# Attention and two feed-forward stages: scores four groups ahead, value spans in two transfers, first weights split in smaller parts

## The chip, the cores and the metric

The kernel runs on one core of a Trainium2 chip. The metric is the device time of one execution in microseconds (us); three runs of the kernel before gave a median of 616.96 us (616.08 to 617.96). The engines are TensorE (PE, its weight loads PEld), VectorE (DVE), ScalarE (ACT), GpSimd (POOL) and SyncE (SP), which issues nearly all transfers (DMA).

## The reference, cut to what matters

```python
# attention, B=2, H=8, S=768, D=64, block 32, band 16
k_sum = k.reshape(B, H, nb, 32, D).max(axis=3)
v_sum = v.reshape(B, H, nb, 32, D).mean(axis=3)
scores_l = where(|i - j| < 16, q @ k.T / sqrt(D), -1e9)
scores_s = q @ k_sum.T / sqrt(D) + log(32)
a = softmax(concat([scores_l, scores_s]))         # sum + 1e-9
x = a @ concat([v, v_sum])                        # -> 1536 tokens x 512
# two feed-forward stages, 512 -> 2048 -> 512
h = maximum(x @ w_in, 0);  x = (h * h) @ w_out
h = x @ w2_in;  g = P(h) / (Q(h) + 1e-6);  out = g @ w2_out
```

## The kernel before, in words

**Attention.** The 16 heads are 8 pairs (`NB`), and a pair's 768 queries are 12 windows of 64 queries, each with 96 keys and 24 block maxima (120 columns, `COLS`). Four windows of both heads make a group, so there are 24 groups G, three to a pair. A group goes through: `scores(G)` on PE; `masked(G)` on DVE (mask and row minimum, from PSUM into a buffer `prob`); `exps(G)` on ACT; `guard(G)` and `invert(G)` on DVE; `normalise(G)` on POOL; `turn(G)` on PE (transpose); a copy to `probT` on ACT; `output(G)` on PE. There are three `prob` buffers (`P_RING`), and PE runs the scores three groups ahead of the output. After every second group DVE splits the result into a high and a low part (`x_hi`, `x_lo`), since every product of the feed-forward stages is three products of such parts.

**Inputs of a pair.** q, kT (padded to 800 columns) and the value windows `vw` (96 rows of 12 x 128 numbers, 6 KB a row) come by one transfer each into rings of three buffers (`RING`). `block_max` on DVE makes the block maxima of the keys in three parts, one a group; POOL builds the key windows (`load_windows`, `spread_all`). `summary(n)` on PE makes the block means of the values, ACT copies them (`copy_summary`), and then SP spreads them by four small transfers into the rows 96 to 119 of the value windows (`spread_summary`); `output(3n)` waits for these.

**What sets the order.** Each engine runs one list written out by hand, with semaphores between them. SP issues in program order: a transfer that has to wait holds up all behind it. Before, iteration n of SP's loop issues the values of pair n+2, k and q of pair n+3 and a first weight slot, and then waits for the summary of pair n+1 (made on PE in group 3n) and spreads it.

**From attention to the first feed-forward stage.** The stage has 48 steps; a step is `hidden` (12 matmuls) and `sum_b` (12 matmuls), with `hidden` two steps ahead. `hidden(0)` and `hidden(1)` stand between the last groups, ahead of `output(22)` and `output(23)`. Their weights (three slots land early) have to be split first: slots 0 and 1 whole on DVE (`split`, after groups 22 and 23's softmax work), slot 2 by halves on POOL, beginning in group 20. Then come the second half of that stage and stage two (`chunk_c`), whose lists the change leaves alone.

Of the kernel before, what the change touches and what calls it, by code (L numbers as in the profile page):

```python
# [28 lines left out]
P = 128  # L29
# [25 lines left out]
DVE_FIRST = 2  # L55
# [6 lines left out]
P_RING = 3  # L62
RING = 3
NB = PAIRS * B
XPAIRS = GROUPS // 2
KP = S + 2 * BAND

# [11 lines left out]
def build(nc, qT, kT, vw, w1, w2, coef_a, coef_b, out):  # L79
# [50 lines left out]
    ksum = [places[1](f"ksum{r}", [P, NBLK]) for r in range(RING)]  # L130
    assert all(a.offset <= w + 2 * half for a, w in zip(places, (W_HI, W_LO)))
    area = Area(WORK)
    prob = [area(f"prob{i}", [P, GU, COLS]) for i in range(P_RING)]
    probT = [area(f"probT{i}", [COLS, GU * P]) for i in range(2)]
    mask = area("mask", [P, 3, COLS])
# [28 lines left out]

    q_in = [sem(f"q_in{r}") for r in range(RING)]
    k_in = [sem(f"k_in{r}") for r in range(RING)]
    vw_in = [sem(f"vw_in{r}") for r in range(RING)]
    vsum_in = [sem(f"vsum_in{r}") for r in range(RING)]
# [7 lines left out]
    means_done = sem("means_done")  # L176
# [24 lines left out]
    w_early, w_late = sem("w_early"), sem("w_late")  # L201
# [27 lines left out]
    def _(sp):  # L229
        def load_k(n):  # L230
            if n >= RING:
                sp.wait_ge(windows_ready, GPB * (n - RING + 1))
            sp.dma_start(kraw[n % RING][:, :], kT[n]).then_inc(k_in[n % RING], 16)
# [6 lines left out]
        def load_vwin(n):  # L240
            if n >= RING:
                sp.wait_ge(o_done, done(2, GPB * (n - RING + 1) - 1))
            sp.dma_start(vwin[n % RING][0:KW, :, :], vw[n]).then_inc(vw_in[n % RING], 16)

        def spread_summary(n):

            sp.wait_ge(vsum_copied, n + 1)
            for t in range(4):
                rows = KW + 2 * GPB * t
                sp.dma_start(vwin[n % RING][rows:rows + 2 * GPB, :, :],  # L250
                             vsum[n % 2][32 * t:32 * t + 2 * GPB, :].unsqueeze(1).to_broadcast([2 * GPB, NW, P])
                             ).then_inc(vsum_in[n % RING], 16)
# [17 lines left out]
        sp.dma_start(ca[:, :], coef_a.partition_broadcast(P)).then_inc(coef_in, 16)  # L270
        sp.dma_start(braw[:, :], coef_b.partition_broadcast(P)).then_inc(coef_in, 16)
        spread_summary(0)
        for n in range(NB):
            if n + 2 < NB:
                load_vwin(n + 2)
            if n + RING < NB:
                load_k(n + RING)
                load_q(n + RING)
            if 2 <= n < 2 + EARLY:
                load_first(n - 2)  # L280
            if n >= 5:
# [24 lines left out]
    def _(pool):  # L306
# [31 lines left out]
        def load_windows(n):  # L338

            pool.wait_ge(k_in[n % RING], 16 * (n // RING + 1))  # L340
# [30 lines left out]
        pool.wait_ge(k_in[0], 16)  # L371
        for gi in range(GPB):
            windows(0, GU * gi, GU * (gi + 1))
# [5 lines left out]
        spread_all(1)  # L379

        for G in range(GROUPS):
            n, gi = divmod(G, GPB)
            if G + 1 < GROUPS:
                normalise(G + 1, (G + 1) % P_RING)
            if n + 2 < NB:
# [4 lines left out]
            x = G - GROUPS + 4  # L390
            if x >= 0:
                if x == 0:
                    pool.wait_ge(w_first, 16 * EARLY)
                if x < 2 * (EARLY - DVE_FIRST):
                    split(half_slot(DVE_FIRST + x // 2, x % 2), w_hi_pool, x, w_early)

# [18 lines left out]
        for x in range(2 * LATE):  # L415
# [4 lines left out]
            split(half_slot(j, x % 2), w_hi_pool, 2 * (EARLY - DVE_FIRST) + x, w_late)  # L420
# [9 lines left out]
    def _(pe):  # L430
# [22 lines left out]
        def summary(n):  # L453

            pe.wait_ge(vw_in[n % RING], 16 * (n // RING + 1))
            pe.wait_ge(vsum_copied, n)
            for j in range(GPB):
                for t in range(4):
                    last = mm(vps[32 * t:32 * t + 32, 0:P], means[:, j, :], vwin[n % RING][0:KW, GPB * t + j, :],  # L459
# [11 lines left out]
        def output(G):  # L471
# [4 lines left out]
            if gi == 0:  # L476
                pe.wait_ge(vsum_in[r], 64 * (n // RING + 1))
# [515 lines left out]
```

## Time and profile before

| | us |
|---|---|
| median of 3 runs | 616.96 (616.08 to 617.96) |
| the profiled execution | 617.14 |
| its span, first to last instruction | 615.4 |
| PE busy | 582.0 (95%) |
| DVE busy | 444.0 (72%) |
| ACT busy | 261.3 (42%) |
| POOL busy | 145.1 (24%) |

The profiled execution lies 0.18 us above the median; 1.74 us of it lie around the span. Busy times are unions over an engine's instructions. The page cuts the span into 40 slices of 15.4 us: attention fills the first five, and the feed-forward stages all that follow.

### The profile page before, as it was taken

What the parts mean: (1) busy time and instruction counts of PE and PEld (TensorE: products, weight loads), DVE (VectorE), ACT (ScalarE), POOL (GpSimd) and SP (SyncE); (2) the same over time, 40 slices, a digit from 0 to 9 for tenths busy, and PEclk for the clock granted to TensorE, in tenths of its full rate; (3) what the DMA queues carried; (4) which work ended last, traced back from release to release, by engine and by line L of the source; (5) the groups of instructions that cost most, each with busy time, mean ns of one, the idle gap of its engine ahead of it and who ended that gap; (6) DMA issues with size and microseconds to landing.
All of it is one profiled execution on the core that took longest, in us unless ns stands there. A gap on an engine that the chain in (4) does not pass through costs nothing.

```text
span 615.4 us, 9725 instructions
## 1 busy us (share of the span) xinstructions
PE 582.0 (95%) x3360; PEld 472.8 (77%) x3360; DVE 444.0 (72%) x834; ACT 261.3 (42%) x553; POOL 145.1 (24%) x150
## 2 busy tenths in 40 slices
PE   4788699999999999999999989999999999999995
PEld 3556578888888888888888867788888888888884
DVE  4678787665343233456675699999999999999996
ACT  3778611111031111311111855556766566766564
POOL 5556610000030000210000656522221222221220
PEclk9999999999999999999999999999999999999999
DMA  8788433000000000022333200000100000100001
GB/s 232 212 261 251 129 128 148 0 1 0 1 0 0 0 0 0 0 81 91 103 102 103 69 1 0 1 0 1 68 0 0 0 0 0 68 1 0 1 2 68
DMA packets 12351, 32.68 MB, mean 53 GB/s; under 512 B 1568, under 2 KB 3872, under 8 KB 12320
## 3 DMA queue, kind: packets, MB, share of 16 engines
q1 hardware_dynamic: 12320, 32.25, 16.8%
q8 instruction: 21, 0.34, 0.2%
q14 instruction: 10, 0.08, 0.0%
HBM read 27.92 MB, written 3.15 MB: 50 GB/s over the span
## 4 chain that ended last, share of the span: by engine, by line
PE 47%; DVE 36%; issue 9%; ACT 3%; DMA 2%; DVEq 1%; POOL 1%; SPq 1%; POOLq 0%
PE bank L499 22%; PE bank L544 21%; DVE ratio L927 9%; DVE numer L909 6%; DVE ratio L921 5%; DVE numer L907 5%; DVE ratio L916 5%; DVE hhi L934 4%; ACT prob L617 2%; DMA vwin<-vsum 2%; PE bank L468 1%; PE bank L449 1%; PE bank L485 1%; PE bank L459 1%; SPq L250 1%
## 5 line engine op out<-in xcount | busy, mean ns | idle before, releaser
L499 PE MATMUL bank<-xhi,whi 128*128 (+1 forms) x384 | 150.3, 391 | 0.3 <-DVE wlo L820 0.3
L499 PE MATMUL bank<-xlo,whi 128*128 (+1 forms) x384 | 149.9, 390 | 0.0
L499 PE MATMUL bank<-xhi,wlo 128*128 (+1 forms) x384 | 149.8, 390 | 0.0
L630 ACT ACTIVATE hsq<-bank 128x512 f32<-128x512 f32 x48 | 28.8, 600 | 218.5 <-PE bank L499 218.5
L409 POOL TENSOR_TENSOR denom<-denom,habs 128x512 f32<-128x512 f32 (+1 forms) x49 | 62.3, 1272 | 250.9 <-ACT denom L686 250.9
L499 PEld LDWEIGHTS bank<-xhi,whi 128*128 128x128 f32 x384 | 72.5, 189 | 15.9 <-DVE wlo L820 0.7
L499 PEld LDWEIGHTS bank<-xhi,wlo 128*128 128x128 f32 x384 | 72.3, 188 | 15.1
L499 PEld LDWEIGHTS bank<-xlo,whi 128*128 128x128 f32 x384 | 72.4, 189 | 14.9
L559 PE MATMUL bank<-whi,hhi 128*128 128x512 f32 x192 | 75.9, 395 | 7.6 <-DVE hlo L938 7.6
L559 PE MATMUL bank<-whi,hlo 128*128 128x512 f32 x192 | 74.8, 390 | 0.0
L559 PE MATMUL bank<-wlo,hhi 128*128 128x512 f32 x192 | 74.8, 389 | 0.0
L544 PE MATMUL bank<-hhi,whi 128*128 128x512 f32 x192 | 74.7, 389 | 0.0
L544 PE MATMUL bank<-hlo,whi 128*128 128x512 f32 x192 | 74.7, 389 | 0.0
L544 PE MATMUL bank<-hhi,wlo 128*128 128x512 f32 x192 | 74.7, 389 | 0.0
L830 DVE TENSOR_TENSOR hsq<-hsq 128x512 f32<-128x512 f32 x48 | 33.5, 698 | 50.0 <-ACT hsq L630 49.8
L833 DVE TENSOR_SCALAR hhi<-hsq 128x512 fp32r<-128x512 f32 x48 | 21.1, 439 | 64.5 <-PE bank L544 64.3
L927 DVE SCALAR_TENSOR_TENSOR ratio<-numer,ca,ratio 128x512 f32<-128x512 f32 (+1 forms) x49 | 56.7, 1157 | 5.7
L401 POOL TENSOR_TENSOR xlo<-xraw,xhi 128x512 fp32r<-128x512 f32 x12 | 17.4, 1484 | 173.4 <-ACT xraw L663 173.4
L683 ACT ACTIVATE habs<-bank 128x512 f32<-128x512 f32 x48 | 28.8, 599 | 66.8 <-PE bank L499 51.6
L559 PEld LDWEIGHTS bank<-whi,hhi 128*128 128x128 f32 x192 | 36.0, 188 | 19.0 <-DVE hlo L938 11.8
L694 ACT ACTIVATE bank<-denom,one 128x512 f32<-128x512 f32 (+1 forms) x49 | 33.6, 686 | 32.3 <-POOL denom L409 32.3
L938 DVE TENSOR_TENSOR hlo<-ratio,hhi 128x512 fp32r<-128x512 f32 (+1 forms) x49 | 42.0, 858 | 1.7
(65 smaller groups left out, 858.9 us busy)
## 6 DMA issues: line engine op xcount, KB each, us to landing
wraw<-w SPq DMA_DIRECT2D x32, 512.0 KB, 4.1
vwin<-vw SPq DMA_DIRECT2D x8, 576.0 KB, 5.4
kraw<-kT SPq DMA_DIRECT2D x8, 400.0 KB, 6.0
q<-qT SPq DMA_DIRECT2D x8, 384.0 KB, 6.4
out<-osb SPq DMA_DIRECT2D x12, 256.0 KB, 2.1
vwin<-vsum SPq DMA_DIRECT2D x32, 36.0 KB
ca<-coef_a SPq DMA_DIRECT2D x1, 2.0 KB, 10.7
braw<-coef_b SPq DMA_DIRECT2D x1, 1.0 KB, 11.8
```

Source lines behind the costliest of these rows:

```text
L409: g.tensor_tensor(denom[:, i, cols], denom[:, i, cols], habs[:, i, cols], ALU.mult).then_inc(q_done, 1)
L499: last = mm(hps[j % 2][:, :], W[a][:, j, kt * P:(kt + 1) * P], X[b][:, kt, bass.ds(CH * c, CH)], start=k == 0, stop=k == 3 * KT - 1)
L544: last = mm(acc[dt][:, :], W[a][:, j, KT * P + dt * P:KT * P + (dt + 1) * P], HID[b][:, j % 2, :], start=j == 0 and i == 0, stop=j == FT - ...
L559: last = mm(acc[t][:, :], HID[a][:, j % 2, t * P:(t + 1) * P], W[b][:, j, KT * P:], start=j == 0 and i == 0, stop=j == FT - 1 and i == 2)
L694: a.activation(rcp0[bank][:, cols], denom[:, i, cols], ACT.Ln, bias=one[:, 0:1]).then_inc(ln_done, 1)
L830: d.tensor_tensor(hsq[:, i, :], hsq[:, i, :], hsq[:, i, :], ALU.mult).then_inc(sq_done, 1)
L907: d.tensor_tensor(numer[:, i, :], hps[i][:, :], numer[:, i, :], ALU.mult).then_inc(horner_done, 1)
L909: d.scalar_tensor_tensor(numer[:, i, :], numer[:, i, :], ca[:, 1:2], hps[i][:, :], ALU.subtract, ALU.mult).then_inc(h_free, 1)
L916: d.scalar_tensor_tensor(ratio[:, cols], denom[:, i, cols], one[:, 0:1], rcp0[bank][:, cols], ALU.add, ALU.mult).then_inc(t1_done, 1)
L921: d.scalar_tensor_tensor(ratio[:, cols], ratio[:, cols], -2.0, rcp0[bank][:, cols], ALU.add, ALU.mult).then_inc(t2_done, 1)
L927: d.scalar_tensor_tensor(ratio[:, cols], numer[:, i, cols], ca[:, 0:1], ratio[:, cols], ALU.subtract, ALU.mult).then_inc(ratio_done, 1)
L938: d.tensor_tensor(hlo[:, i, cols], ratio[:, cols], hhi[:, i, cols].bitcast(F32), ALU.subtract).then_inc(g_ready, 1)
```

## The change

- **Look-ahead.** Four `prob` buffers; PE runs the scores four groups ahead, ACT the exponentials three, DVE `guard` and `invert` and POOL `normalise` two groups ahead of `turn`, one more than before at each.
- **Values.** Four value buffers (`V_RING`); each value load is two transfers of 96 rows of 3 KB. `summary(n)` stands in group 3n-4 for n from 3 on, and in groups 0, 1 and 3 for n = 0, 1 and 2. SP's iteration n loads pair n+3 whole and then spreads pair n+2; ahead of the first spread it now also loads the values of pair 2 and the keys of pair 3.
- **Start.** The keys of pair 0 come in three parts, one of them issued by ACT; keys are no longer padded in memory, the edges are cleared on DVE; the copies that make `means` go from DVE to ACT.
- **First weights.** The w_in half of slots 0 to 2 is split on POOL in six quarter slots, one in each of the groups 17 to 22; the w_out half on DVE in groups 21 to 23. PE does `hidden(0)` and `hidden(1)` in eight pieces of three matmuls, two in each of the groups 20 to 23.

SP's list, pairs 1 to 3, before. `vwin<-vw` is a value load, `vwin<-vsum` a spread, `kraw` keys, `wraw` a weight slot; the numbers in the names are buffers.

```order
L250 DMA vwin_69<-vsum_75 6x12x128 x4
L243 DMA vwin_65<-vw 96x1536
L233 DMA kraw_67<-kT 128x800
L238 DMA q_66<-qT 128x768
L250 DMA vwin_73<-vsum_74 6x12x128 x4
L243 DMA vwin_69<-vw 96x1536
L233 DMA kraw_71<-kT 128x800
```

SP's list at the same keys (`kraw_67` of pair 4, `kraw_71` of pair 5), now.

```order
L240 DMA kraw_67<-kT 128x768
L249 DMA q_66<-qT 128x768
L262 DMA vwin_73<-vsum_74 6x12x128 x4
L262 DMA vwin_85<-vsum_75 6x12x128 x4
L255 DMA vwin_69<-vw 96x768 x2
L240 DMA kraw_71<-kT 128x768
```

The keys of pair 5 stood behind the spread of pair 2; now they stand behind that of pair 3, whose summary PE makes in group 5. The keys of pairs 6 and 7 likewise stand behind the spreads of pairs 4 and 5 (summaries in groups 8 and 11).

PE's list in the last four groups, before: `bank<-ident,prob` is `turn`, `bank<-probT,vwin` is `output`, `bank<-xhi,whi` the first matmul of `hidden`.

```order
L468 MATMUL bank<-ident,prob_81 120x128 x4
L485 MATMUL bank<-probT_82,vwin_69 64x64 x8
L468 MATMUL bank<-ident,prob_79 120x128 x4
L485 MATMUL bank<-probT_83,vwin_69 64x64 x8
L468 MATMUL bank<-ident,prob_80 120x128 x4
L499 MATMUL bank<-xhi,whi 128x512
L499 MATMUL bank<-xlo,whi 128x512
L499 MATMUL bank<-xhi,wlo 128x512
```

PE's list in group 20 and at the head of group 21, now.

```order
L502 MATMUL bank<-ident,prob_79 120x128 x4
L533 MATMUL bank<-xhi,whi 128x512
L533 MATMUL bank<-xlo,whi 128x512
L533 MATMUL bank<-xhi,wlo 128x512
L533 MATMUL bank<-xhi,whi 128x512
L533 MATMUL bank<-xlo,whi 128x512
L533 MATMUL bank<-xhi,wlo 128x512
L519 MATMUL bank<-probT_83,vwin_73 64x64 x8
L502 MATMUL bank<-ident,prob_80 120x128 x4
```

Before, the first matmul of `hidden` came in group 22 and all 12 together; now six stand in each of the four groups between `turn` and `output`.

```diff
-DVE_FIRST = 2
-P_RING = 3
+P_RING = 4
+V_RING = 4
+THIRD = S // GPB
+SPLIT_FROM = GROUPS - 7
+SUMMARY_AT = [0, 1, 3] + [GPB * n - 4 for n in range(3, NB)]
...
         def load_vwin(n):
-            if n >= RING:
-                sp.wait_ge(o_done, done(2, GPB * (n - RING + 1) - 1))
-            sp.dma_start(vwin[n % RING][0:KW, :, :], vw[n]).then_inc(vw_in[n % RING], 16)
+            if n >= V_RING:
+                sp.wait_ge(o_done, done(2, GPB * (n - V_RING + 1) - 1))
+            for half in (slice(0, NW // 2), slice(NW // 2, NW)):
+                sp.dma_start(vwin[n % V_RING][0:KW, half, :], vw[n][:, half, :]).then_inc(vw_in[n % V_RING], 16)
...
-        load_k(0)
+        load_k_first(0)
+        load_k_first(2)
         load_q(0)
+        load_vwin(0)
         load_k(1)
-        load_vwin(0)
         load_q(1)
+        load_k(2)
         load_vwin(1)
-        load_k(2)
         load_q(2)
-        spread_summary(0)
         for n in range(NB):
-            if n + 2 < NB:
-                load_vwin(n + 2)
+            if n == 0:
+                load_vwin(2)
+            elif n + RING < NB:
+                load_vwin(n + RING)
             if n + RING < NB:
                 load_k(n + RING)
+            if n == 0:
+                spread_summary(0)
+                load_vwin(RING)
+                spread_summary(1)
+            if n + RING < NB:
                 load_q(n + RING)
             if 2 <= n < 2 + EARLY:
                 load_first(n - 2)
...
-            if n + 1 < NB:
-                spread_summary(n + 1)
+            if n == 1:
+                spread_summary(2)
+            if 0 < n and n + 2 < NB:
+                spread_summary(n + 2)
...
+        def split_in(x):
+            j, part = x // 2, SLOT // 4 * (x % 2)
+            index = slice(None), j, slice(part, part + SLOT // 4)
+            split(index, w_hi_pool, x, w_in_ready)
...
-            if G + 1 < GROUPS:
-                normalise(G + 1, (G + 1) % P_RING)
+            if G + 2 < GROUPS:
+                normalise(G + 2, (G + 2) % P_RING)
...
+        early = {GROUPS - 4: [(0, 0), (0, 1)], GROUPS - 3: [(0, 2), (1, 0)],
+                 GROUPS - 2: [(0, 3), (1, 1)], GROUPS - 1: [(1, 2), (1, 3)]}
...
         for G in range(GROUPS):
             turn(G, G % P_RING)
-            if G + P_RING < GROUPS:
-                scores(G + P_RING)
-            if G % GPB == 0 and G // GPB + 1 < NB:
-                summary(G // GPB + 1)
...
+            for ahead in (3, 4) if G == 0 else (4,):
+                if G + ahead < GROUPS:
+                    scores(G + ahead)
+            for n in range(1, NB):
+                if SUMMARY_AT[n] == G:
+                    summary(n)
+            for j, kt in early.get(G, ()):
+                hidden_first(j, kt)
             output(G)
...
-            if G + 2 < GROUPS:
-                exps(G + 2, (G + 2) % P_RING)
+            if G + 3 < GROUPS:
+                exps(G + 3, (G + 3) % P_RING)
...
         for G in range(GROUPS):
-            if G + 1 < GROUPS:
-                guard(G + 1)
+            if G + 2 < GROUPS:
+                guard(G + 2)
+                invert(G + 2)
             if G >= 2:
                 (x_lo if G % 2 else x_hi)(G // 2 - 1)
-            if G + 1 < GROUPS:
-                invert(G + 1)
...
+            for n in range(3, NB):
+                part = G - GPB * (n - 2) + 1
+                if 0 <= part < GPB:
+                    block_max(n, part, 1)
+            for ahead in (3, 4) if G == 0 else (4,):
+                if G + ahead < GROUPS:
+                    masked(G + ahead)
+            if G >= GROUPS - EARLY:
+                split_out(G - GROUPS + EARLY)
```

`block_max` of pair n still begins in DVE's group 3n-7 (keys of pair 5 in group 8), as before.

## Rows read from the trace of the kernel before

**Rows 1.** The page: busy tenths of PE, granted clock, 40 slices.
```profile
PE   4788699999999999999999989999999999999995
PEclk9999999999999999999999999999999999999999
```

**Rows 2.** Chain of waits, 30 to 44 us: start, length, what.
```profile
36.54 5.67 DMA vwin<-vsum
```

**Rows 3.** Timeline of PE in attention: start, length, instructions, idle time before.
```profile
12.26 1.08 PE L449 MATMUL bank<-kwin,q 64*64 64x120 f32 x16
...
18.46 0.69 PE L485 MATMUL bank<-probT,vwin 120*64 120x64 f32 x16 [1.64 <-issue]
19.07 0.65 PE L468 MATMUL bank<-ident,prob 128*120 128x128 f32 x4
19.66 0.64 PE L449 MATMUL bank<-kwin,q 64*64 64x120 f32 x16
...
25.02 0.86 PE L459 MATMUL bank<-vwin,means 96*32 96x128 f32 x24
25.81 0.69 PE L485 MATMUL bank<-probT,vwin 120*64 120x64 f32 x16
...
28.89 0.65 PE L468 MATMUL bank<-ident,prob 128*120 128x128 f32 x4 [0.45 <-POOL prob L359]
...
68.25 0.65 PE L468 MATMUL bank<-ident,prob 128*120 128x128 f32 x4
```

**Rows 4.** Chain of waits, 62 to 90 us.
```profile
61.88 0.99 POOL prob L359
...
69.00 0.56 ACT probT L638
69.57 1.53 ACT prob L617 x8
...
73.56 1.90 DVE wlo L820
...
75.51 4.29 PE bank L499 x12
...
87.31 2.72 PE bank L544 x12
```

**Rows 5.** Windows: us, busy by engine, granted clock, DMA share, GB/s.
```profile
6.00:15.00 9.00, 5.85 (x92) 4.48 (x88) 4.08 (x29) 3.99 (x19) 4.09 (x10) 1.00 1.01 254
15.00:17.00 2.00, 1.82 (x32) 0.99 (x26) 0.94 (x5) 1.63 (x10) 1.63 (x2) 1.00 0.56 122
18.00:22.00 4.00, 3.44 (x72) 2.76 (x72) 1.21 (x11) 2.24 (x10) 1.38 (x2) 1.00 1.00 319
75.00:78.00 3.00, 2.67 (x7) 2.01 (x7) 2.96 (x6) 0.59 (x1) 2.92 (x3) 0.50 0.00 0
```

**Rows 6.** Timeline of SP: start, length of issue, transfer.
```profile
26.84 3.07 SPq L250 DMA_DIRECT2D vwin<-vsum  x4
...
30.95 0.34 SPq L243 DMA_DIRECT2D vwin<-vw  x1
31.33 0.42 SPq L233 DMA_DIRECT2D kraw<-kT  x1
```

**Rows 7.** Time to landing of that key load, issued at 31.33 us.
```profile
DMA to landing us min/median/max: 5.5/5.5/5.5
```

**Rows 8.** Timeline of DVE: `block_max` of pair 5; one of a group's four `masked`.
```profile
37.38 0.39 DVE L770 TENSOR_REDUCE ksum<-kraw 128x8 f32<-128x256 f32 x1
...
70.07 0.27 DVE L786 CUSTOM_DVE_ANT_0 prob<-bank,mask 128x120 f32<-128x120 f32 x1
```

**Rows 9.** Timeline of POOL at the end of attention.
```profile
71.71 1.27 POOL L369 TENSOR_TENSOR wlo<-wraw,whi 128x512 fp32r<-128x512 f32 x1
72.94 1.43 POOL L359 TENSOR_TENSOR prob<-prob,inverse 128x480 f32<-128x480 f32 x1
```

**Rows 10.** Timeline of ACT: a copy of summaries.
```profile
12.39 0.27 ACT L625 COPY vsum<-bank 128x128 f32<-128x128 f32 x1 [2.72 <-PE bank L459]
```

More of the change, by code:

```diff
@@ L491, in _, with hidden @@
         W, X, HID = (whi, wlo), (xhi, xlo), (hhi, hlo)
-        def hidden(c, j, n):
-            pe.wait_ge(h_free, done(2, n - 2))
-            k = 0
-            for kt in range(KT):
-                for a, b in PARTS:
+        def hidden(c, j, n, kts=range(KT)):
+            if kts[0] == 0:
+                pe.wait_ge(h_free, done(2, n - 2))
+            for kt in kts:
+                for i, (a, b) in enumerate(PARTS):
                     last = mm(hps[j % 2][:, :], W[a][:, j, kt * P:(kt + 1) * P],
-                              X[b][:, kt, bass.ds(CH * c, CH)], start=k == 0, stop=k == 3 * KT - 1)
-                    k += 1
-            last.then_inc(h_full, 1)
+                              X[b][:, kt, bass.ds(CH * c, CH)], start=kt == 0 and i == 0, stop=kt == KT - 1 and i == 2)
+            if kts[-1] == KT - 1:
+                last.then_inc(h_full, 1)
         def weights_ready(index):
-            if index < DVE_FIRST:
-                pe.wait_ge(w_ready, index + 1)
-            elif index < EARLY:
-                pe.wait_ge(w_early, 2 * (index - DVE_FIRST + 1))
+            if index < EARLY:
+                pe.wait_ge(w_in_ready, 2 * (index + 1))
             elif index >= 2 * FT - LATE:
@@ L611, in _ @@
             act.sem_inc(out_written[t], 16)
+        act.dma_start(kraw[0][:, BAND + THIRD:BAND + 2 * THIRD], kT[0][:, THIRD:2 * THIRD]).then_inc(k_first[1], 16)
+        a.preload_act_table_set("natural_log_exp_and_others")
+        act.wait_ge(consts, 3)
+        act.wait_ge(means_clear, 1)
+        for j in range(GPB):
+            last = a.copy(means[:, j, 2 * j:2 * j + 2], mean[:, :])
+        last.then_inc(means_done, 1)
         def exps(G, r):
@@ L736, in _ @@
         dve.sem_inc(g_ready, 2)
+        for r in range(RING):
+            d.memset(kraw[r][:, 0:BAND], 0.0)
+            last = d.memset(kraw[r][:, BAND + S:], 0.0)
+        last.then_inc(edges, 1)
+        d.memset(means[:, :, :], 0.0).then_inc(means_clear, 1)
         d.memset(one[:, :], 1.0 + 1e-6).then_inc(coef_step, 1)
@@ L750, in make_mask @@
             d.memset(mask[QW:P, 2, KW - BAND:KW], MASKED).then_inc(mask_step, 1)
[L752 to L759 removed]
         def block_max(n, part, parts):
             r = n % RING
[L764 to L765 removed]
+            if n == 0:
+                dve.wait_ge(k_first[part], 16)
+            elif part == 0:
+                dve.wait_ge(k_in[r], 16 * (n // RING + (r > 0)))
                 if n >= RING:
@@ L835, in square, with split_out @@
             d.tensor_tensor(hlo[:, i, :], hsq[:, i, :], hhi[:, i, :].bitcast(F32), ALU.subtract).then_inc(g_ready, 1)
+        def split_out(j):
+            raw, hi, lo = (t[:, j, KT * P:] for t in (wraw, whi, wlo))
+            dve.wait_ge(w_first, 16 * EARLY)
+            d.tensor_scalar(hi, raw, 1.0, None, ALU.mult).then_inc(w_out_hi, 1)
+            dve.wait_ge(w_out_hi, j + 1)
+            d.tensor_tensor(lo, raw, hi.bitcast(F32), ALU.subtract).then_inc(w_out_ready, 1)
         make_mask()
-        block_max(0, 0, GPB)
-        make_means()
+        for part in range(GPB):
+            block_max(0, part, 1)
         masked(0)
-        block_max(1, 0, GPB)
         masked(1)
```

135 lines of the change are left out of this document (67 added, 68 removed).

## The prediction

> **What bounds the kernel now.** I read the slices of the page first [rows 1]. From the sixth slice on PE is at 9 tenths or more in nearly every slice at the full clock, and the change touches nothing of what runs there. In the first five it stands at 4, 7, 8, 8 and 6. So all that the change can give or take lies between the start and the first `sum_b`, which begins at 87.3 us [rows 4]; whatever happens before it shifts the rest as a block. The shift of that matmul is what I work out.
>
> Next I read PE's timeline, the chain and the transfers in that stretch. The first `output` starts at 18.46 us; `output(3)`, the first of the second pair, at 25.81, 7.35 us later; `turn(20)` at 68.25, 42.44 us after that; and the first `sum_b` 18.9 us (to the start of its row in the timeline, 87.15) to 19.1 us (by the chain, 87.31) after `turn(20)` [rows 3, 4]. I take 18.9. The middle part is 17 groups and runs at 2.5 us a group. What an engine needs is less: ACT copies in 0.56 us and takes its exponentials in 1.53, which with the 0.02 between is 2.11 us a group [rows 4]. The difference is waiting: for a spread of summaries, which lands 5.67 us after its last issue [rows 2], and for the loop copy, exponentials, normalise, turn.
>
> **The start: a longer transfer queue before the first spread.** Before, 3 key loads of 400 KB, 3 of q of 384 and 2 of values of 576 KB stood ahead of the first spread, 3504 KB. Now it is 4 x 384 + 3 x 384 + 3 x 576 = 4416 KB, 912 KB (0.93 MB) more. The transfer engines were full there: a share of 1.01 at 254 GB/s from 6 to 15 us, and 1.00 at 319 from 18 to 22 [rows 5]. So it costs 3.7 or 2.9 us, 3.3 in the middle. From 15 to 17 us the share was only 0.56 [rows 5], since that queue was running dry; behind it now stands more work, which gives 0.9 us back: +2.4 us for the first `output`. It would be nothing or even a gain (down to -2.5 us, since the summary itself is made earlier) if the small transfers did not queue behind the large ones, and +3.7 us at most. The Trainium skill says that on each transfer engine descriptors are consumed in ring order (DMA: Bandwidth & Descriptors, Queues, rings and completion order); by that the spread does queue, and the row's 5.67 us for so small a transfer [rows 2] agrees.
>
> **Output(0) to output(3).** The spread of pair 1 now hangs on a summary made in group 1. After `output(0)` starts: itself 0.62 us, `turn(1)` 0.60, `scores(5)` 0.57, `summary(1)` 0.79 (pitches of the later rows in [rows 3]); then ACT finishes `exps(4)` and copies, 1.1 us; four issues, 3.07 us [rows 6]; and a landing of 1.5 us, an estimate (the nearest row, 5.67, is a full queue; here it is empty). Sum 8.25 us against 7.35: +0.9. (ACT's share is what is left of `exps(4)` when the summary ends, 0.8, and the copy, 0.27 [rows 10].) But PE will have stood idle for 5 us before it, and rows after an idle start are slow: the same 16 scores took 1.08 us at 12.3 us and 0.64 at 19.7 [rows 3]. With all four steps longer by that ratio, 2.58 us become 4.4, ACT then needs only 0.3, and it is 9.3 us, +2.0. I take +1.8, with 0.9 and 2.7 (a landing of 2.2) as ends. The Trainium skill holds that throttled is the array's default state and activity releases it (TensorE: Matmul & The Clock Gate, What's actually happening); by that the sum has 2.0 here, and without it 0.9. The granted clock of this stretch is written as 1.00, so the record does not confirm it there, but the durations do.
>
> **Output(3) to turn(20).** With the look-ahead one group deeper, `normalise` is done a group early, and its wait in front of `turn` (0.45 us in [rows 3]) goes. What is late next is ACT: three groups of 2.11 and a copy of summaries, 0.27 [rows 10], are 6.6 us a pair, against 7.5 before. So 0.6 us and 16 groups x 2.2 = 35.8 us.
>
> To this comes a wait that is new. SP must finish a spread before it issues the keys of the pair after. Before, the keys of pair 5 were issued at 31.33 us, 2.4 us after `turn(5)` at 28.89, landed 5.5 us on, at 36.8, and DVE used them at 37.38 [rows 3, 6 to 8]: 0.5 us to spare. Now the spread of pair 3 is in the way, whose summary is made in group 5: copied 3.05 us after `turn(5)` (0.65 turn, 0.5 copy, 1.6 exponentials, 0.3), four issues 3.07, two value issues 0.8: the keys are issued 6.95 us after `turn(5)` and land at +12.05 to +12.45; I take 5.1 us from issue, since the first value half was issued 0.35 us earlier relative to them than in the row. DVE wants them at +8.5. Behind the waiting `block_max` (0.39) stand `masked(12)` (0.85, four of the second of [rows 8] at a pitch of some 0.21) and, on ACT, `exps(12)` (1.6), the copy for `output(10)` (0.64) and that output (0.62): `turn(11)` comes at +16.15 where six groups of 2.2 would give +13.2. That is 2.95 us. The keys of pair 6 are asked for after the spread of pair 4, which this wait doesn't delay, so they are nearly in time (0.3); pair 7 pays 2.95 again. Together 6.2: 42.0 us against 42.4, -0.4 us. Ends: no such waits -6.6, waits of 3 us in all four batches (pairs 4 to 7) +5.4.
>
> The value load in two transfers costs SP one more issue of 0.34 us, counted above. The Trainium skill states that larger transfers saturate the memory better and advises to batch 2 KB into 4 or 8 (Perfetto Trace Analysis, DMA Optimizations); by that halving the rows speaks against this change. No row separates row sizes. If the 0.59 MB of a pair's values moved at 254 instead of 319 GB/s it would be 0.47 us on each key landing and about +1 us in the sum; without it, 0.
>
> **The end of attention.** Before, 18.9 us. They hold four turns (0.60 each), four outputs (0.62) and 36 matmuls of `hidden` (2.72 us for 12, the row of 12 in [rows 4]), 13.1 us of work. The rest is DVE's whole-slot splits ahead of `hidden(0)` (1.90 us for the low part alone), POOL's half-slot splits ahead of `normalise`, and the half clock: granted 0.50 from 75 to 78 us, by which `hidden(0)` took 4.29 us in place of 2.72 [rows 4, 5, 9]. Now POOL splits a quarter slot a group from group 17 on: half of a half slot's work, about 1.0 us beside 0.99 of `normalise` [rows 4], in 2.11; PE fills the wait between turn and output with six matmuls (1.36 us), and its clock has no reason to fall. With four turns, four outputs and three hiddens back to back and 0.1 of gaps I get 13.2: -5.7 us. If POOL's two operations run at their slow rate (1.43 and 1.27 [rows 9]) it falls a group behind: -4.2.
>
> **Sum.** +2.4 +1.8 -0.4 -5.7 = -1.9 us. The profiled execution took 617.14 (615.4 of span and 1.74 around it), so 615.2; it lies 0.18 above the median of 616.96, and the forecast against that is 615.1 us. The edges of k cleared on DVE, `means` on ACT and the keys of pair 0 in thirds I cost at nothing: the first scores wait for all three parts of `block_max`, which DVE cannot begin before its mask is made, and DVE and ACT then wait for the first output anyway; uncovered they would be 0.5 us.
>
> **Rivals.**
> - *The keys come in time, or the start doesn't slip.* For it: the 0.5 us to spare shows that the landing is close, and the deeper look-ahead may swallow more of a wait than I allow. Against: SP's order alone makes the key issue 4.5 us later (6.95 against 2.44 after `turn(5)`). Without the two long waits it is -1.9 - 5.8 = -7.7, 609.2 us; with an unchanged start as well -11.5, 605.5 us.
> - *Slower: the loop spread, keys, block_max, summary closes on every pair.* One mechanism at SP's in-order list: four waits of 3 us make the middle part +5.4 and the sum +2.4 +1.8 +5.4 -5.7 = +3.9, 620.9 us. It decides once the waits for keys sum to more than 8.1 us (5.7 - 2.4 - 1.8 = 1.5 above the 6.6 that the deeper look-ahead gives), that is from the third long one. Against: pair 4's keys stand behind no late spread.
> - *The end pays less.* POOL falls behind, and the half clock comes back in a wait for weights: -5.7 becomes about -2, the sum +1.8, 618.8 us.
>
> **How the numbers follow.** Differences under 0.3% (1.85 us) count as no change. The forecast's case gets 0.45, with a range of its own of 612 to 618.5; the rival with keys in time 0.33; the closed loop 0.15; the weak end 0.07. Faster: 0.33 and somewhat under half of the first case, 0.22, is 0.55; no change: 0.19 of the first case and 0.01; slower: 0.04 of it, 0.15 and 0.06. The range 607.5 to 619.5 leaves out the full gain and the whole closed loop.
>
> **What would show it.** The first `output` near 21 us; PE idle for some 5 us before it and slow rows after; `output(3)` near 30; waits of DVE's `ksum` on `kraw<-kT` of 3 to 4 us for pairs 5 and 7; `normalise` no longer ending a wait of PE; `turn(20)` near 72; no clock of 0.50 near 75 us, and the first `sum_b` near 85.3, after which all goes as before. I am wrong if DVE never waits for keys (then it is faster), if it waits four times, or if the spread lands out of the queue's order.

## The result, and the profile of the changed kernel

The changed kernel takes 621.47 us (median of 8 runs, 619.3 to 625.11) against 617.73 for the kernel before (8 runs, 616.08 to 621.43): ratio 1.0066, 95% interval [1.0035, 1.0097]. Two more measurements gave 1.0041 [1.0019, 1.0062] (10 runs) and 1.0066 [1.0036, 1.0097] (12 runs). It is slower: the medians of the three measurements lie 3.7, 2.4 and 4.8 us above those of the kernel before. Forecast were 615.1 us and a range up to 619.5. Its profiled execution took 619.3 us with a span of 617.2, the shortest of the eight.

Busy slices of PE and the granted clock, of the page; they stand against [rows 1]:

```profile
PE   4587899999999999999999989999999999999995
PEclk9999999999999999999999999999999999999999
```

From the sixth slice on all is as before: from the first `sum_b` to the end it is 528.3 us here and in both traces of before. (Attention itself reaches into the sixth slice, up to that matmul.) In this trace the whole difference lies before it; in the third measurement's trace the end took 529.4 us, so 1.1 us lie behind it. PE's timeline of that stretch (start, length, instructions, idle time before), against [rows 3]:

```profile
12.93 1.88 PE L483 MATMUL bank<-kwin,q 64*64 64x120 f32 x32
22.04 1.12 PE L519 MATMUL bank<-probT,vwin 120*64 120x64 f32 x16 [7.23 <-issue]
23.09 1.11 PE L502 MATMUL bank<-ident,prob 128*120 128x128 f32 x4
24.13 1.08 PE L483 MATMUL bank<-kwin,q 64*64 64x120 f32 x16
25.14 1.28 PE L493 MATMUL bank<-vwin,means 96*32 96x128 f32 x24
...
32.34 0.69 PE L519 MATMUL bank<-probT,vwin 120*64 120x64 f32 x16 [1.42 <-DMA vwin<-vsum]
...
34.90 0.65 PE L502 MATMUL bank<-ident,prob 128*120 128x128 f32 x4
...
39.92 0.69 PE L519 MATMUL bank<-probT,vwin 120*64 120x64 f32 x16 [1.24 <-issue]
...
50.41 0.69 PE L519 MATMUL bank<-probT,vwin 120*64 120x64 f32 x16 [1.39 <-ACT probT L687]
51.03 0.65 PE L502 MATMUL bank<-ident,prob 128*120 128x128 f32 x4
...
75.36 0.65 PE L502 MATMUL bank<-ident,prob 128*120 128x128 f32 x4
...
88.91 0.39 PE L585 MATMUL bank<-hhi,whi 128*128 128x512 f32 x1
```

The starts of `output(0)`, `output(3)`, `turn(20)` and the first `sum_b` cut it as the forecast does. The last two columns are the traces of the same kernel in its second and third measurement; the column of before is from [rows 3] and the first `sum_b`'s row at 87.15.

| | before | after, forecast | after | again | third |
|---|---|---|---|---|---|
| start to `output(0)` | 18.46 | +2.4 | 22.04 (+3.6) | 21.10 (+2.6) | 21.49 (+3.0) |
| to `output(3)` | 7.35 | +1.8 | 10.30 (+3.0) | 10.41 (+3.1) | 10.54 (+3.2) |
| to `turn(20)` | 42.44 | -0.4 | 43.02 (+0.6) | 45.24 (+2.8) | 45.53 (+3.1) |
| to the first `sum_b` | 18.90 | -5.7 | 13.55 (-5.35) | 13.55 | 13.57 |
| sum | 87.15 | -1.9 | 88.91 (+1.8) | 90.30 (+3.2) | 91.13 (+4.0) |

Three terms cost more than forecast and one gives a little less. The first trace shows the changed kernel at its best, with the clock at 1.00 in every stretch of 20 us of attention; the other two executions, of 620.76 and 622.64 us, lie at the medians of their measurements. The second trace of the kernel before (experiment 7) has its first `sum_b` at 86.01, so the column of before is itself uncertain by about 1 us.

### The profile page after: what moved, and what is told of

It reads as the page before. It is cut to its first block, busy times and chain, and to the rows that moved or that the text cites. A ratio compares the mean times of both kernels' runs of the same rounds, so it can differ in the third digit from the quotient of the medians.

```text
span 617.2 us, 9768 instructions
## 1 busy us (share of the span) xinstructions
PE 581.2 (94%) x3360; PEld 473.0 (77%) x3360; DVE 443.0 (72%) x839; ACT 261.6 (42%) x556; POOL 147.2 (24%) x158
## 3 DMA queue, kind: packets, MB, share of 16 engines
q1 hardware_dynamic: 13360, 31.99, 16.1%
## 4 chain that ended last, share of the span: by engine, by line
PE 46%; DVE 35%; issue 9%; ACT 3%; DMA 3%; SPq 2%; DVEq 1%; POOL 0%; POOLq 0%
PE bank L533 22%; PE bank L585 21%; DVE ratio L981 9%; DVE numer L963 6%; DVE ratio L975 5%; DVE numer L961 5%; DVE ratio L970 5%; DVE hhi L988 4%; DMA kraw<-kT 3%; ACT prob L665 2%; SPq L262 1%; PE bank L502 1%; PE bank L519 1%; DVE hlo L992 1%; PE bank L483 1%
```

## What the trace of the changed kernel shows

**The start.** A window over the wait for the first spread (us, busy by engine, granted clock, DMA share, GB/s), against [rows 5], and SP's issues, against [rows 6]:

```profile
12.00:20.00 8.00, 2.69 (x36) 1.94 (x34) 4.50 (x24) 3.12 (x15) 4.90 (x7) 1.00 1.06 240
```

```profile
11.49 3.27 SPq L262 DMA_DIRECT2D vwin<-vsum  x4
...
26.79 3.06 SPq L262 DMA_DIRECT2D vwin<-vsum  x4
...
40.98 0.91 SPq L255 DMA_DIRECT2D vwin<-vw  x2
41.94 0.43 SPq L240 DMA_DIRECT2D kraw<-kT  x1
...
45.51 3.07 SPq L262 DMA_DIRECT2D vwin<-vsum  x4
48.62 1.34 SPq L255 DMA_DIRECT2D vwin<-vw  x2
50.01 0.43 SPq L240 DMA_DIRECT2D kraw<-kT  x1
```

The spread's last issue ends at 14.76 and `output(0)` starts at 22.04, 7.3 us later. The transfer engines are full (a share of 1.03 to 1.11) until 20 us, and at 0.58 in the last two.

**The keys.** DVE's timeline, the four `block_max` that wait, for the keys of pairs 4 to 7:

```profile
37.69 0.42 DVE L818 TENSOR_REDUCE ksum<-kraw 128x8 f32<-128x256 f32 x1 [0.95 <-DMA kraw<-kT]
...
47.01 0.42 DVE L818 TENSOR_REDUCE ksum<-kraw 128x8 f32<-128x256 f32 x1 [2.68 <-DMA kraw<-kT]
...
55.40 0.42 DVE L818 TENSOR_REDUCE ksum<-kraw 128x8 f32<-128x256 f32 x1 [2.18 <-DMA kraw<-kT]
...
64.14 0.42 DVE L818 TENSOR_REDUCE ksum<-kraw 128x8 f32<-128x256 f32 x1 [2.55 <-DMA kraw<-kT]
```

Pair 4's keys were taken to be in time ("stand behind no late spread"). They stand behind the spread of pair 1, which is late itself (issued at 26.79, the keys at 31.32), and DVE waits 0.95 us. For pair 5 the forecast holds step for step: `turn(5)` at 34.90, keys issued 7.04 us later (forecast 6.95) and landed 12.1 us later (12.05 to 12.45), `turn(11)` at 51.03, 16.1 us later (16.15). For pair 6 it does not. Its keys were to be 0.3 us late; they were issued at 50.01 and DVE stood 2.18 us. The spread of pair 4 ahead of them was issued at 45.51, because PE had first stood 1.24 us before `output(6)`, for the spread of pair 2, which comes late too. With 0.43 us more for the value issues in front (1.34 against 0.91) and 0.3 us more to landing, that is the difference. `turn(14)` comes at 59.42, 8.39 us after `turn(11)`, where the forecast has 6.9.

From 14 to 98 us PE has no wait for `normalise` left, as forecast; in the trace of before they sum to 6.4 us there.

**The clock.** In the other traces of the same kernel it falls where PE waits for these keys. The third measurement's trace, windows and PE's timeline:

```profile
50.00:52.00 2.00, 1.85 (x20) 1.64 (x20) 1.97 (x13) 1.63 (x9) 1.96 (x4) 0.50 1.03 309
52.00:54.00 2.00, 2.00 (x34) 1.41 (x36) 0.91 (x5) 1.65 (x8) 0.99 (x1) 0.50 1.01 316
54.00:56.00 2.00, 2.00 (x33) 1.48 (x26) 1.21 (x10) 0.72 (x4) 0.00 (x0) 0.50 0.73 289
```

```profile
50.15 1.12 PE L519 MATMUL bank<-probT,vwin 120*64 120x64 f32 x16 [1.39 <-ACT probT L687]
51.20 1.11 PE L502 MATMUL bank<-ident,prob 128*120 128x128 f32 x4
...
55.74 1.11 PE L502 MATMUL bank<-ident,prob 128*120 128x128 f32 x4
56.78 0.64 PE L483 MATMUL bank<-kwin,q 64*64 64x120 f32 x16
```

PE waited 1.39 us before `output(10)` here as in the first trace. Here it then worked at 0.50 (1.2 GHz), with rows of 1.1 us where 0.65 stood: `output(10)` to `output(12)` took 7.37 us against 5.37 (50.15 to 57.52, and 50.41 to 55.78). It is the same wait with and without a fall of the clock behind it.

## The experiments

My theory after the result: each of the forecast's four mechanisms is there, three come out dearer than I had them, and the clock may add to the waits. Rivals: that 3 KB rows are slower, and that the new end of attention doesn't pay in the time. All edits are to the changed kernel unless said.

**1. The first spread earlier in SP's list.**

```diff
             if n == 0:
+                spread_summary(0)
                 load_vwin(2)
...
             if n == 0:
-                spread_summary(0)
                 load_vwin(RING)
```

> The changed kernel, with the values of pair 2 and the keys of pair 3 issued behind the first spread instead of ahead of it. Theory A (the transfer list: the change lost its gain in SP's order): the first output starts near 18.8 us instead of 22.04, PE's idle time before it is 4 us instead of 7.2, and the first sum_b moves from 88.9 to about 86; the span is some 3 us below that of the changed kernel (617.2), the ratio to the kernel before about 1.002. Theory B (the start is covered by the waits for keys that follow): the first output moves, the first sum_b stays at 88 to 89. Theory C (most of the 4 us in the median is TensorE's clock falling in the idle start): the mean granted clock of the timed runs rises above 0.996 and their spread shrinks.

Measured: 616.95 us, ratio 0.9977 [0.9947, 1.0007], that is 0.6 to 0.9% under the changed kernel (1.0041 and 1.0066). PE's timeline:

```profile
17.10 1.12 PE L519 MATMUL bank<-probT,vwin 120*64 120x64 f32 x16 [2.06 <-issue]
```

Two loads (0.98 MB) taken out of the way move `output(0)` from 22.04 to 17.10. `output(0)` to `output(3)` stays at 10.48, so that term has a cause of its own. The first `sum_b` starts at 87.14 where I expected 86: the middle part took 46.01, with the clock at 0.83 from 40 to 80 us.

**2. The keys ahead of the spread.** Keys of pair n+4 are issued ahead of the spread of pair n+2.

```diff
-            if n + RING < NB:
-                load_k(n + RING)
...
+            if n + 1 + RING < NB:
+                load_k(n + 1 + RING)
```

> The changed kernel, with the keys of pair n+4 issued ahead of the spread of pair n+2 instead of behind it. Theory A: DVE's waits for keys (8.4 us in all in the changed kernel) fall under 1.5 us, output(3) to turn(20) takes 37 to 38 us instead of 43.0, the first sum_b comes at about 83.5, the span is 5 to 5.5 us shorter, the ratio to the kernel before 0.997 to 0.999. Theory B (the middle part is bound by the bytes of the transfers, 2 MB a pair): the waits move from the keys to q, the values or the spreads and the middle part stays above 41 us. Theory C (clock): no change in the median beyond the span's.

Measured: 620.67 us, 1.0035 [1.0009, 1.006]. The trace has a span of 613.0. DVE's waits from 14 to 98 us (us in total, times, longest), of the changed kernel and then of this one:

```profile
DVE ksum L818 <- DMA kraw<-kT: 8.4, 4, 2.7
```

```profile
DVE ksum L820 <- DMA kraw<-kT: 0.5, 1, 0.5
```

The waits for keys go, and `output(3)` to `turn(20)` falls from 43.02 to 38.36: 4.7 us, at a clock of 1.00 in both. By the ratios the gain over the changed kernel is only 0.4 to 1.9 us, with intervals that overlap, and 1.0035 is not the 0.997 to 0.999 that I expected. So I ran it once more.

> The changed kernel with the keys ahead of the spreads, once more. Its first trace had a span 4.2 us under the changed kernel's, but its median was only 1.7 us under. Theory C: the trace was one with hardly any fall of the clock (0.997); others lose it in the idle start or at the head of stage two, so a second trace shows a granted clock below 1 somewhere and the first sum_b between 83.6 and 87. Theory A alone would give the first sum_b within 0.5 us of 83.6 in every trace.

Measured: 619.84 us, 1.0026 [0.9997, 1.0055]. The first `sum_b` starts at 90.80, outside the 83.6 to 87 that I expected. Here the same part took 43.34 us, in which the clock stood at 0.91 from 40 to 60 us and 0.83 from 60 to 80. Part of it is a stop of PE of 2.86 us that I had not expected (last section), and slow rows stand behind this stop and behind the wait before `output(6)`. How much the other executions lose in this way, two traces don't tell: the mean granted clock of all executions of this kernel, 0.991 to 0.992, is about that of the changed kernel (0.991 to 0.994). What is left besides is a wait of PE for a spread (2.4 us before `output(6)` in both traces).

**3. Both edits.**

> Both edits of SP's list together. Theory A: the gains add, first output near 18.8, first sum_b at 80 to 81, span about 609, ratio to the kernel before 0.988 to 0.993. If the bytes of the transfers bind (B), not under 0.997.

Measured: 616.64 us, 0.994 [0.9909, 0.997]; first `sum_b` at 83.15. SP's order alone turns the changed kernel from 0.4 to 0.7% slower into 0.6% faster than before. The two gains don't simply add: `output(0)` starts at 16.93, but the middle part takes 42.23, not the 38.36 of experiment 2. In it DVE still waits 3.52 us for the keys of pair 7, and PE 2.15 us before `output(6)`, with slow rows behind that wait.

**4. Values by one transfer.**

```diff
-            for half in (slice(0, NW // 2), slice(NW // 2, NW)):
-                sp.dma_start(vwin[n % V_RING][0:KW, half, :], vw[n][:, half, :])...
+            sp.dma_start(vwin[n % V_RING][0:KW, :, :], vw[n])...
```

> The changed kernel, with each value load as one transfer of 6 KB rows again. Theory A: two transfers cost SP 0.35 us of issue ahead of each key load and nothing else, so the keys land 0.3 to 0.5 us earlier in each of two or three waits: 0 to 1.5 us faster than the changed kernel, ratio to the kernel before 1.004 to 1.007. Rival (3 KB rows move slower than 6 KB rows): more than 2 us faster, the first output at 21 us or earlier. Opposite rival (3 KB rows help): slower than the changed kernel by 1 us or more.

Measured: 622.23 us, 1.0061 [1.0031, 1.0091], where the changed kernel has 1.0041 to 1.0066: the split of the value loads costs and gives nothing that can be told from the noise. The intervals leave room for some 2 us either way, so the 1 us that the forecast estimated is not excluded. Its parts are 20.68, 10.29, 45.17 and 14.03, close to those of the changed kernel. `output(0)` at 20.68 is a sign that I had given to the rival, but it lies only 0.4 us under the earliest of the changed kernel's three, which differ by 0.9.

**5. The end of attention as before.** The early `hidden` pieces and the quarter-slot splits undone, the rest kept.

```diff
-        early = {GROUPS - 4: [(0, 0), (0, 1)], GROUPS - 3: [(0, 2), (1, 0)], ...
+            j = G - GROUPS + 2
+            if j >= 0:
+                weights_ready(j)
```

> The changed kernel with the end of attention as before (whole and half slots split, hidden(0) and hidden(1) whole in groups 22 and 23). Theory A: the 5.4 us that the new end gives go back, since it is the only term of the sum that came out as forecast: turn(20) at 75 us as in the changed kernel, the first sum_b near 94, span 622 to 623 in a trace without a fall of the clock, ratio to the kernel before 1.013 to 1.018. Rival (the new end only ends a wait that would have ended anyway, or the clock pays for it): less than 3 us slower than the changed kernel.

Measured: 627.03 us (4 runs), 1.0166 [1.0104, 1.0227]. `turn(20)` to the first `sum_b` is 18.64 us, against 13.55. PE's timeline shows what had gone:

```profile
81.84 0.80 PE L528 MATMUL bank<-xhi,whi 128*128 128x512 f32 x1 [2.17 <-DVE wlo L855]
82.43 0.63 PE L528 MATMUL bank<-xlo,whi 128*128 128x512 f32 x1
```

A wait for DVE's split, then matmuls at 0.63 that take 0.39 at the full clock. The new end is worth 5.1 us in the trace. By the ratios it is 6 to 8 us, from four executions; the interval lies clear of those of the changed kernel.

**6. SP's list of before.** Three value buffers, one transfer each, summaries and SP's order as before; look-ahead and new end kept.

```diff
-V_RING = 4
-SUMMARY_AT = [0, 1, 3] + [GPB * n - 4 for n in range(3, NB)]
+V_RING = 3
+SUMMARY_AT = [0] + [GPB * (n - 1) for n in range(1, NB)]
```

> The changed kernel with SP's list, the three value buffers, the single value transfer and the places of the summaries all as before; look-ahead, start on the other engines and new end stay. Theory A (the loss is in the list alone): first output at 18.5, no waits of DVE for keys beyond 2 us, waits of 1 to 3 us for spreads in two or three pairs, turn(20) at 66 to 68, first sum_b at 79.5 to 81.5, ratio to the kernel before 0.986 to 0.992. Rival (the deeper look-ahead itself costs): first sum_b at 84 or later, ratio above 0.996.

Measured: 613.77 us (7 runs), 0.9935 [0.9906, 0.9964]; parts 19.61, 8.71, 41.22, 13.52. PE waits twice in the middle, for spreads:

```profile
43.81 0.69 PE L509 MATMUL bank<-probT,vwin 120*64 120x64 f32 x16 [2.14 <-DMA vwin<-vsum]
...
59.27 0.73 PE L509 MATMUL bank<-probT,vwin 120*64 120x64 f32 x16 [2.32 <-DMA vwin<-vsum]
```

This is the change without its new order of transfers, and it is 0.65% faster than before. The new order, with the value buffers and the places of the summaries that go with it, turns that into 0.4 to 0.7% slower: about 7 us (6.5 to 8 by the ratios). The trace lies between my two theories: the first `sum_b` is at 83.06, later than the 79.5 to 81.5 of theory A and earlier than the 84 of the rival. Against the trace of before its parts are +1.15, +1.4, -1.2 and -5.4, so nearly all it gains is the new end. The 1.15 us at the start are about as much as `output(0)` varies between traces of one kernel.

**7. Both kernels once more**, for the spread between executions.

> The changed kernel once more, on the same chip and with the same runs of the kernel before as the two others. Theory A gives a ratio of 1.003 (the 1.8 us of the two traces) plus what the clock adds; the measured 1.0066 says 1.0035 to 1.0097. The trace shows whether the first sum_b stays at 88.9 us and whether the granted clock falls in the waits for keys, which the first trace didn't show (clock 0.999).

> The kernel before once more, for a second trace: the first sum_b at 87.2 us within 1 us if the order of waits is steady, later by up to 3 us if the clock falls in attention. The length from the first sum_b to the end is 528.3 us in the first trace; a fall of the clock in stage two would add to it.

Measured: 620.74 us, 1.0041 [1.0019, 1.0062] for the changed kernel, parts in the table above. The kernel before gave one run of 616.05 with parts 18.14, 7.76, 41.50, 18.61, so its first `sum_b` starts at 86.01, 1.1 us earlier than in the first trace.

**8. Summaries a group earlier.** On top of 3: summaries of pairs 1 and 2 in groups 0 and 2, the spread of pair 2 ahead of the values of pair 4.

```diff
-SUMMARY_AT = [0, 1, 3] + ...
+SUMMARY_AT = [0, 0, 2] + ...
```

> Both edits of SP's list (first spread ahead of the later loads, keys ahead of spreads), and the summaries of pairs 1 and 2 in groups 0 and 2 instead of 1 and 3, so that the spread of pair 1 no longer hangs on the first output. Theory A: first output at 17, output(3) 7.5 to 8 us later instead of 10.4, turn(20) 38 to 39 us after that, the end 13.6: first sum_b at 76 to 78, ratio to the kernel before 0.980 to 0.988. Rival (the transfer queue then makes output(3) or output(6) late anyway): no better than both edits alone, 0.994.

Measured: 614.34 us, 0.9947 [0.9921, 0.9972], no better than both edits alone (0.994), as the rival has it, and far from the 0.980 to 0.988 that I expected. `output(0)` to `output(3)` falls from 10.44 to 8.35, but `output(0)` starts 1.05 us later in this trace, so `output(3)` comes only 1.0 us earlier, and 0.6 us in experiment 10, which has the same list. The middle part takes 41.51, not 38 to 39: in it PE waits for keys and a spread (1.04 and 1.06 us) and stops for 1.76 us (last section). The first `sum_b` is at 81.49, the earliest of all traces, but not at 76 to 78.

**9. The same with PE kept busy at the start**, by 17 transposes of the identity into a bank that nothing reads yet (ten at the very start, three ahead of the first turn, four ahead of `output(0)`).

> The same kernel (e8_summaries_early) with 17 additional transposes of the identity into a free bank, in PE's idle stretches at the start (10 ahead of the first scores, 3 and 4 in the gaps before the first output). Theory C (idle stretches cost by the clock): the first output's 16 matmuls take 0.69 us instead of 1.12 and the rows to output(3) shrink, the first sum_b comes 1 to 2 us earlier. If the slow rows are not the clock, nothing or up to 1 us slower.

Measured: 613.25 us (6 runs), 0.9922 [0.9893, 0.9952]. Its interval overlaps that of 8; in its trace the slow rows only came one group later (`output(1)` at 1.12 in place of `turn(1)` at 1.11). The row that I had named as the sign, `output(0)` at 0.69, was at 0.69 in experiment 8 already, and the first `sum_b` came 1.7 us later (83.15), behind three stops of PE. Whether the transposes give anything here is not settled. By the ratio this is the fastest kernel of all, but its interval also overlaps that of experiment 6.

**10. Look-ahead of three groups** and three `prob` buffers, otherwise as 8.

```diff
-P_RING = 4
+P_RING = 3
```

> The same kernel (e8_summaries_early) with the look-ahead back at three groups and three prob buffers. Theory A: the wait of turn for normalise is back, 0.3 to 0.8 us a group in most groups, output(3) to turn(20) takes 41.5 to 43 us instead of 38.4, so it is 3 to 5 us slower than e8. Rival (the deeper look-ahead gives nothing once the list is mended, ACT binds either way): within 1.5 us of e8.

Measured: 615.78 us, 0.9961 [0.9935, 0.9986], against 0.9947 [0.9921, 0.9972]: by the medians the deeper look-ahead gives 1.4 us, which the intervals don't separate from nothing. That is the rival's "within 1.5 us", not the 3 to 5 us of theory A. The trace has the waits for `normalise` again, this one the longest, but also the stop of PE of the last section:

```profile
49.33 0.65 PE L504 MATMUL bank<-ident,prob 128*120 128x128 f32 x4 [1.50 <-POOL prob L384]
```

**11. The waits kept, PE busy in them.** The changed kernel with 25 transposes ahead of `output(0)` and 6 each ahead of `output(10)`, `(13)` and `(16)` (`warm` issues that many transposes of the identity), beside the changed kernel on the same chip.

```diff
+            if G == 0:
+                warm(ops[1][:, 0:P], 25)
+            if G in (10, 13, 16):
+                pe.wait_ge(vsum_copied, (G + 5) // 3)
+                warm(vps[:, P:2 * P], 6)
```

> The changed kernel with PE's long waits in attention filled: 25 transposes of the identity into a bank that nothing reads yet ahead of output(0), and six each, into the unused columns of the summary bank, ahead of output(10), output(13) and output(16), where PE waits for the late key loads. Nothing that is waited for gets earlier. Theory that a part of the 4 us is TensorE's clock, which falls after these waits: the matmuls of output(0) take 0.69 us in place of 1.12, the granted clock stays at 1.00, output(0) to output(3) takes about 9.5 us in place of 10.3 to 10.4, the first sum_b starts at 88 to 89 us, and the median lies about 2 us under that of the changed kernel (ratio to before 1.003 or less). Rival, that all of it is waiting for transfers: no stretch shortens, the ratio stays at 1.004 to 1.007, or grows by up to 2 us where the transposes outlast a wait.

> The changed kernel once more, on the same chip as the one with filled waits: 619 to 622 us, ratio 1.004 to 1.007; the first sum_b at 88.9 to 90.5 us by how often the clock falls in the waits.

Measured: 619.58 us, 1.0024 [1.0002, 1.0046], against 622.68 us, 1.0066 [1.0036, 1.0097]. The first `sum_b` of the changed kernel's new trace starts at 91.13, later than the 88.9 to 90.5 that I expected. Over the 12 runs of each the means differ by 3.0 us (resampled, 1.4 to 4.6 in 95 of 100). PE's timeline:

```profile
14.49 4.63 PE L558 MATMUL bank<-ident 128*128 128x128 f32 x25
20.64 0.69 PE L519 MATMUL bank<-probT,vwin 120*64 120x64 f32 x16 [1.52 <-issue]
21.26 0.65 PE L502 MATMUL bank<-ident,prob 128*120 128x128 f32 x4
```

Useless work takes 3 us off the time: `output(0)` and what follows run at 0.69, 0.65 and 0.64 in place of 1.12, 1.11 and 1.08, `output(0)` to `output(3)` takes 9.04 us in place of 10.3 to 10.5, `output(3)` to `turn(20)` 42.56, as in the first trace at the full clock (43.02), and the clock is 1.00 in every stretch of 20 us up to 340 us. DVE waits for keys as before (8.0 us in all). The first `sum_b` starts at 85.79, earlier than the 88 to 89 I expected: 1.4 us of it are `output(0)` at 20.64, which varies by as much between traces of one kernel (22.04, 21.10, 21.49). So some 3 us of the changed kernel's time are the clock's answer to its idle stretches. They can't simply be taken off the 7 us of the new order: the kernels that they are compared with lose by the clock too (see what stays open).

## Why the prediction was wrong

**Start, +2.4; measured +3.6, +2.6 and +3.0.** The mechanism is right, as experiment 1 shows (22.04 to 17.10 by order alone). The 0.93 MB moved at 240 GB/s, the rate of 12 to 20 us, take 3.9 us, not the 3.3 I took from the rates of [rows 5]; less the 0.9 of idle queue that is 3.0, the middle of the three. My upper end of 3.7 held. The Trainium skill says that the descriptors on each transfer engine are consumed in ring order (DMA: Bandwidth & Descriptors, Queues, rings and completion order); that the spread lands late behind the loads and early ahead of them, at 22.04 and 17.10, agrees with it.

**`output(0)` to `output(3)`, +1.8; measured +3.0 to +3.2.** Slow rows after the idle stretch were forecast, and the four of them end at 26.4, as I had it (4.4 us after `output(0)`). What was too small is the landing. By the chain it took 3.08 us from the start of the last issue, so `output(3)` began 2.5 us after the issue's end, where I put 1.5, with 2.2 as the upper end. The queue was as empty as I had assumed:

```profile
26.00:28.00 2.00, 2.00 (x50) 1.52 (x40) 1.62 (x8) 0.95 (x4) 0.99 (x1) 1.00 0.01 4
28.00:30.00 2.00, 1.90 (x44) 1.37 (x36) 1.17 (x11) 2.00 (x10) 0.00 (x0) 1.00 0.23 50
```

```profile
29.13 3.08 DMA vwin<-vsum
```

The windows show a DMA share of 0.01 and 0.23: the four small transfers needed this long with the queue nearly empty (2.97 us in experiment 11), and I had set it 1 us too low without a row. Experiment 11 also gives the price of the slow rows, 1.3 us by 10.3 against 9.04. What the place of the summary makes is less clear: `output(3)` comes 0.6 to 1.0 us earlier in experiments 8 and 10 than in 3.

**`output(3)` to `turn(20)`, -0.4; measured +0.6, +2.8 and +3.1. This is the step that failed**, and in two places. The sentence that the keys of pair 6 are nearly in time, since "this wait doesn't delay" the spread of pair 4, was wrong: another did. I had not followed `output(6)`, which stands for the spread of pair 2 (1.24 us), and all of SP's later steps with it. There were three long waits for keys and a short one for pair 4's, not two.

From `turn(5)` to `turn(11)` the forecast holds to 0.02 us (16.13 against 16.15); from `turn(11)` to `turn(14)` it is 1.5 us short. The waits for keys were not too cheap in all: experiment 2 gives their price at the full clock as 4.7 us, while the wait before `output(6)` grew by 1.2, so 5.9, where I had 6.2. What my sum lacked is the wait for the spread of pair 2, a term that I had at nothing: 35.8 of work, 5.9 and 1.24 make 42.9, against the 43.02 of the first trace and my 42.0.

Second, I had priced waits at the full clock. In two of three traces the clock fell to 0.50 behind the waits at `output(10)` and `output(16)`, and this part took 2.2 and 2.5 us more. The rows for it stood before me: [rows 5] has the half clock at 75 us after a wait, and I used it for the end of attention but not for the waits that the change adds.

**End of attention, -5.7; measured -5.35.** Right: `hidden` fills PE's waits, and the row of 75 to 78 us, 0.50 in [rows 5], is at 1.00. Experiment 5 brings back both the wait and the slow rows.

**Sum.** -1.9 became +1.8 in the best trace and +3.2 and +4.0 in the others; the 2.4 to 4.8 us of the medians are of this size. Every error went the same way, the first two for causes of their own (the rate of the queue, the landing of a small transfer) and the third through SP's list: a later spread makes a later output, that a later summary and a later spread, and the keys stand behind these. My rival of the closed loop had 0.15, and of the cases named it is the nearest: its point of decision (waits for keys of 8.1 us in all, a third long one) was passed with 8.4 us. That its 620.9 us lie so near the measured 621.47 is in part luck. It has +5.4 in the middle part, where the traces have +0.6 to +3.1, and +4.2 up to `output(3)`, where they have +5.7 to +6.6. One sum among the rivals doesn't come out: with an unchanged start, -7.7 less 2.4 and the 1.1 of slow rows is -11.2 and 605.8 us, not -11.5 and 605.5; nothing hangs on it.

**3 KB rows.** The advice of the Trainium skill to batch small transfers into larger ones (Perfetto Trace Analysis, DMA Optimizations) makes no difference that these runs can show: experiment 4 has 1.0061 with rows of 6 KB, the changed kernel 1.0041 to 1.0066 with 3 KB. A loss of the 1 us that I estimated would not stand out.

**What stays open.** In both traces of before the clock is at 0.91 from 60 to 80 us, and in one at 0.94 from 20 to 40, so that kernel pays for waits too. Over all executions its mean granted clock is 0.991 to 0.992, no higher than the changed kernel's 0.991 to 0.994, and experiment 6 has the lower 0.990. So these runs show what the clock costs the changed kernel (experiment 11, where the mean rises from 0.991 to 0.995), but not that it makes the difference to the kernel before. Why `output(0)` varies by 1 us between traces of one kernel was not tried.

## What to carry to other kernels

Where one engine issues transfers in a fixed order, a step that is moved earlier in that list must be followed through everything behind it, to the next turn of the loop and the one after: the gain was in the new end of attention (5 us), and the new order of transfers took 7. Put the small transfer on which a matmul hangs ahead of the large ones that are needed later. A wait of 1.4 us on TensorE came to 3.4 where the clock fell behind it (2.0 us of slow rows), so price new waits at both clocks, and look at more than one trace before you call a stretch clean.

## What I had not expected of the hardware

PE stopped in the middle of a row of like matmuls, with no semaphore between them. Experiment 2's second trace, PE's timeline and windows:

```profile
70.73 0.63 PE L485 MATMUL bank<-kwin,q 64*64 64x120 f32 x13
74.22 0.66 PE L485 MATMUL bank<-kwin,q 64*64 64x120 f32 x3 [2.86 <-issue]
74.81 1.12 PE L521 MATMUL bank<-probT,vwin 120*64 120x64 f32 x16
```

```profile
70.00:72.00 2.00, 1.35 (x25) 0.89 (x21) 1.61 (x11) 2.00 (x10) 1.60 (x4) 1.00 0.94 368
72.00:74.00 2.00, 0.00 (x0) 0.00 (x0) 0.35 (x1) 0.99 (x6) 1.92 (x3) 0.72 0.78 165
74.00:76.00 2.00, 1.78 (x20) 1.36 (x21) 0.81 (x7) 0.00 (x0) 0.02 (x1) 0.50 0.94 236
```

Thirteen of sixteen scores, 2.86 us of nothing, then three more and rows at half clock. Such stops, of 1.3 to 2.9 us, stand in the traces of experiments 2 (the second), 8, 9 and 10, and in none of the five of before and of the changed kernel. Loads were in flight each time, but not always at a full queue: around the stop of experiment 8 the share was 0.29 and 0.75. What PE waits for there no run tells. But by the record the four traces with such stops are also the four that were taken on one of the three chips (for the very first traces of both kernels none is on record). Experiment 2's first trace, of the same kernel on another chip, has none, and experiment 3, on that other chip too, none above 0.52 us. So the stops may belong to that chip and not to the better orders of transfers; no run separates the two. In the traces that have them they take 1.8 us (experiment 8) to 5.2 us (experiment 9).

The record of the clock can also say 1.00 where rows are slow: the window of 22 to 26 us of the changed kernel's first trace does, and the rows from 22.04 on take 1.1 us where the same ones take 0.65 later:

```profile
22.00:26.00 4.00, 3.96 (x53) 3.16 (x57) 0.54 (x5) 1.76 (x8) 0.00 (x0) 1.00 0.07 23
```
